# First expert chosen at run time, no slots for empty experts, weight chunks and VectorE steps moved: attention, mixture of experts and a dense layer on one core

## What is computed

```python
# attention: q, k, v (8, 8, 576, 64), p (8, 8, 32, 64)
p_packed = sm_attn(p, k, v)
out = sm_attn(q, p_packed, p_packed)
# mixture of experts: N = 4608 tokens, D = 512, E = 8, F = 1024
logits = x @ w_gate
expert_idx = np.argmax(logits, axis=1)
...
for e in range(E):
    mask = expert_idx == e
    if not mask.any():
        continue
    xe = x[mask]
    h = np.maximum(xe @ w1[e], 0.0)
    ye = h @ w2[e]
    out[mask] = gate_w[mask, None] * ye
# dense: 512 -> 2048 -> 512
h = x @ w_in
r = np.maximum(h, 0.0)
g = s * (r * r) + b
return (g @ w_out).astype(np.float32)
```

## Time and profile before

| | |
|---|---|
| three runs | 1541.33 us median (1539.59 to 1544.24) |
| the profiled execution | 1552.85 us, of which 1551.0 us are the span of its trace |
| PE busy | 1459.8 us (94%) |
| DVE, ACT, POOL busy | 31%, 31%, 27% |
| chain that ended last | PE 91%, DVE 3%, issue 3%, ACT 1%, DMA 1%, POOL 1% |
| 24718 instructions | PE 8664, DVE 811, ACT 973, POOL 275 that count as busy |

### The profile page before, as it was taken

How to read it: one execution, slowest core, us unless ns; L and a number is a source line. 1 busy time by engine, 2 the same in 40 slices (tenths; PEclk the granted TensorE clock), 3 DMA queues, 4 the chain that set the end, 5 groups by cost and what they waited for, 6 DMA issues and landing times.

```text
span 1551.0 us, 24718 instructions
## 1 busy us (share of the span) xinstructions
PE 1459.8 (94%) x8664; PEld 1174.4 (76%) x8665; DVE 475.2 (31%) x811; ACT 479.9 (31%) x973; POOL 413.2 (27%) x275
## 2 busy tenths in 40 slices
PE   6887369999999999998999999999999999999996
PEld 5655358888888888886888888888888888888885
DVE  3777621111111111113523232322323232332322
ACT  5666123333333333332222222222222222222221
POOL 1244578448266557104501010100101010010100
PEclk9899579999999999999999999999999999999998
DMA  9798345234243333212101010100101000000000
GB/s 315 219 273 237 117 152 160 84 108 135 68 142 108 108 122 115 81 47 89 63 14 42 7 41 14 35 13 14 41 7 41 14 34 14 14 27 0 27 1 27
DMA packets 52850, 122.78 MB, mean 79 GB/s; under 512 B 6608, under 2 KB 12752, under 8 KB 52816
## 3 DMA queue, kind: packets, MB, share of 16 engines
q1 hardware_dynamic: 33728, 79.21, 16.8%
q10 hardware_dynamic: 13136, 24.19, 5.0%
q0 software_dynamic: 5952, 18.92, 3.4%
HBM read 90.78 MB, written 31.52 MB: 79 GB/s over the span
## 4 chain that ended last, share of the span: by engine, by line
PE 91%; DVE 3%; issue 3%; ACT 1%; DMA 1%; POOL 1%; another core or an unknown queue 0%; ACTq 0%; DVEq 0%
PE psum L675 18%; PE psum L676 18%; PE psum L677 18%; PE psum L751 8%; PE psum L750 8%; PE psum L749 8%; PE psum L719 2%; PE psum L508 2%; PE psum L684 1%; PE psum L737 1%; PE psum L610 1%; PE psum L548 1%; PE psum L569 1%; PE psum L623 1%; DVE x_rows L1142 1%
## 5 line engine op out<-in xcount | busy, mean ns | idle before, releaser
L1256 DVE SCALAR_TENSOR_TENSOR s_r_r<-r_relu,s_col 128x512 f32<-128x512 f32 x144 | 116.1, 806 | 449.3 <-ACT r_relu L973 449.3
L483 POOL DMA_INDIRECT out_dram<-out_sb,out_row_of_y x36 | 35.6, 989 | 746.9 <-ACT out_sb L983 738.7
L675 PE MATMUL psum<-weights_split,gT_hi 128*128 128x512 f32 x576 | 230.9, 401 | 2.3 <-DVE gT_lo L1258 2.2
L973 ACT ACTIVATE r_relu<-psum 128x512 f32<-128x512 f32 x144 | 86.1, 598 | 470.9 <-PE psum L751 456.2
L676 PE MATMUL psum<-weights_split,gT_hi 128*128 128x512 f32 x576 | 227.7, 395 | 0.0
L677 PE MATMUL psum<-weights_split,gT_lo 128*128 128x512 f32 x576 | 227.7, 395 | 0.0
L751 PE MATMUL psum<-yT_hi,weights_split 128*128 128x512 f32 x576 | 227.3, 395 | 0.0
L749 PE MATMUL psum<-yT_hi,weights_split 128*128 128x512 f32 x576 | 225.7, 392 | 0.0
L750 PE MATMUL psum<-yT_lo,weights_split 128*128 128x512 f32 x576 | 225.5, 392 | 0.0
L396 POOL TENSOR_TENSOR weights_split<-weights_raw,one 128x1024 fp32r<-128x1024 f32 x70 | 135.3, 1933 | 253.6 <-PE psum L677 243.1
L398 POOL TENSOR_TENSOR weights_split<-weights_raw,weights_split 128x1024 fp32r<-128x1024 f32 x70 | 169.6, 2423 | 5.5
(11 more groups left out here) (154 smaller groups left out, 1833.3 us busy)
## 6 DMA issues: line engine op xcount, KB each, us to landing
weights_raw<-in_moe_w_dram SPq DMA_DIRECT2D x64, 512.0 KB
x_slot<-x_by_expert ACTq DMA_DIRECT2D x40, 257.0 KB, 2.7
y_sorted<-y_slot ACTq DMA_DIRECT2D x40, 256.5 KB, 3.2
k_sb<-in_k_dram SPq DMA_DIRECT2D x16, 576.0 KB, 6.4
q_sb<-in_q_dram SPq DMA_DIRECT2D x16, 576.0 KB, 7.6
v_sb<-in_v_dram SPq DMA_DIRECT2D x48, 192.0 KB
y_tile<-y_sorted SPq DMA_DIRECT2D x32, 256.5 KB, 2.6
weights_raw<-in_moe_w_in_dram SPq DMA_DIRECT2D x8, 512.0 KB
```

Of the source, the lines that this page charges most:

```text
L675: nc.tensor.matmul(dst, lhs[0][:, col:col + P], rhs[0], start=first_, stop=False)
L973: nc.scalar.activation(rel[:], ps[:, HFB + par, :], ACT.Relu).then_inc(rel_done, 1)
L1256: nc.vector.scalar_tensor_tensor(sq[par][:], rel[:], s_col[:], rel[:], ALU.mult, ALU.mult).then_inc(sq_done, 1)
```

## The change

It has five parts.

- **First expert.** In unit 5 VectorE takes the expert with the most tokens in batch 0 (`lead_expert`; with these inputs expert 3). Its chunks are the first to be loaded, now in units 10 to 15 and behind the last one, and it comes first in the order of slots.
- **Order and empty experts.** The tables first sort the experts: the chosen one, then the others, and those without tokens last. An empty expert has no slot. There are still eight loads of weights; if experts are empty, the last one with slots is loaded again, and its slots are cut between its loads (`starts`, `expert_of`). With these inputs expert 7's ten slots become 5 and 5. The tables now end in two places: `tables` when rows and slot count are there, `wtables` when the weight tables are.
- **Slot 0.** SyncE issues its load, at row 0 of the chosen expert's region, once batches 0 to 5 are scattered (2 x 96 on `x_sent[0]` and `[1]`, on the other two as `lead_count` says: 96 if the chosen expert has 256 tokens in six batches, and it has 576). Its up projection waits neither for tables nor for the last scatters, and VectorE does its `x_lo` ahead of the tables, its `h_lo` behind both. TensorE does slot 0's down projection ahead of slot 1's up.
- **Scatters.** All scatters of batches 6 and 7 now wait for the last positions. GpSimd splits all eight chunks of the second expert.
- **VectorE's last steps** are written out one by one: the `turn_packs` of the last unit goes ahead of `positions` of batch 6, and `experts` of batch 7 ahead of the last two `out_x`.

```diff
             for u in range(2, UNITS):
                 load_k(u)
                 load_q(u)
-                if u % 2 == 0:
-                    n = u // 2 - 1
-                    chunk(n, n, expert_chunk(0, n))
+                if u == UNITS - NCH + 2:
+                    sp.wait_ge(lead_done, 2)
+                    lead_ = sp.value_load(lead_i[0:1, 0:1], min_val=0, max_val=E - 1)
+                    row = sp.value_load(lead_row[0:1, 0:1], min_val=0, max_val=(E - 1) * REG)
+                if u >= UNITS - NCH + 2:
+                    n = u - (UNITS - NCH + 2)
+                    chunk(n, n, expert_chunk(lead_, n))
                 load_v(u)
...
+            for b in range(XBUFS):
+                sp.wait_ge(x_sent[b], 2 * BATCH_DMA if b < 2 else sent)
+            sp.wait_ge(t0_full, UNITS)
+            sp.wait_ge(t1_full, UNITS)
+            sp.dma_start(xin[:], rows_dram[bass.ds(row, P), :]).then_inc(xin_in, 16)
+            sp.wait_ge(wtables, 1)
+            second = sp.value_load(expert_of[0:1, 1:2], min_val=0, max_val=E - 1)
+            for n in range(EARLY, 2 * NCH):
+                chunk(n % NCH, n, expert_chunk(second, n % NCH))
...
-            for j in range(4, J):
+            pool.wait_ge(pos_done, B)
+            for j in range(J):
                 scatter(B - 2, j)
             for j in range(J):
                 scatter(B - 1, j)
 
             for sent in x_sent:
                 pool.wait_ge(sent, BATCH_DMA * B // XBUFS)
-            pool.wait_ge(conv, EARLY + 2)
-            for n in range(EARLY + 2, 2 * NCH):
+            for n in range(EARLY, 2 * NCH):
                 split(n % NCH, n, WBUF)
...
+            x_hi(0)
+            keep_columns(0, 0)
+            act.wait_ge(need_done, 1)
+            sent = act.value_load(sent_need[0:1, 0:1], min_val=BATCH_DMA, max_val=2 * BATCH_DMA)
+            for b in range(XBUFS):
+                act.wait_ge(x_sent[b], 2 * BATCH_DMA if b < 2 else sent)
             act.wait_ge(tables, 1)
...
             load(1)
             relu(0)
+            h_hi(0)
             x_hi(1)
             keep_columns(1, 1)
+            for sent in x_sent:
+                act.wait_ge(sent, 2 * BATCH_DMA)
             load(2)
...
-            step(nc.vector.tensor_scalar(nslot[0][:, 0, E:], cnt_i[:], 1.0, None, ALU.max))
+            step(nc.vector.tensor_copy(nslot[0][:, 0, E:], cnt_i[:]))
```

301 lines of the change are left out of this document (208 added, 93 removed).

## The result

The changed kernel took **1533.72 us** (median of 6 runs, 1527.77 to 1543.43), the kernel before beside it 1542.78 us (1539.59 to 1550.04). The ratio is 0.9931, 95% interval [0.9907, 0.9954]: faster, by 9 to 10.6 us. Forecast were 1521.7 us, a gain of 19.6 and a range of 1509 to 1531. The direction was right; half of the gain did not arrive, and the time lies above the range.

What follows compares the result with a forecast made beforehand. TensorE was taken to bound the expert stage, plus its waits ahead of it. Terms 12.5 + 7.6 - 0.5 = 19.6 us, off the median 1541.3, gave 1521.7 us; range 1509 to 1531.

Steps and rivals of the forecast that it cites:

- One slot fewer, 12.5 us: Expert stage: the empty expert's slot goes, 39 slots in place of 40, gaining 12.5 us.
- Slot 2's up projection 7.6 us earlier: Turn from attention to experts: slot 0's early start brings slot 2's up projection to 221.8 from 229.36, 7.6 us.
- hole ending at 28.7: After slot 0's up projection: TensorE stands some 8 us for VectorE's tables, until the down projection at 206.1.
- Half of the head start is spent on tables: Slot 0's up projection starts 16.3 us earlier, but after waiting for VectorE's tables only 7.6 remain at slot 2.
- Positions of batch 7: VectorE at the end of attention: reordered last steps make these positions end 1.7 us earlier, at 188.6.
- The gap of 4.1 us: VectorE's unexplained late start at 183.76: kept in the path; by bounds 4.1 us gained or 2.2 lost.
- lead_expert, 0.5 us: Attention stage, unit 5: choosing the expert adds seven small VectorE instructions, taken as 0.5 us lost.
- the moved chunks, 0: Attention stage: moving chunk loads to units 10 to 15 taken as nothing, bounds 2.7 us gained and 5 lost.
- Behind 229 us nothing changes but the count of slots.: Everything after slot 2's up projection, including the dense stage: no change assumed except one slot fewer.
- It does not do what it says: Rival, expert stage: the empty expert keeps a slot, 12.5 us more, 1534 us; chance 0.02.
- The head start is spent altogether: Rival, turn to experts: table chains cost over 7 us more, slot 2 no earlier, 1529 us; chance 0.10.
- Slower: Rival, attention units 10 to 15: chunks on full DMA engines cost 28 us, 1550 us; chance 0.03 over 24 us, 0.02 under.

Runs made afterwards that it cites:

- e1: The changed kernel, unedited, run again for a second profile; ratio to the kernel before 0.9935 [0.9921, 0.9949].
- e13: The changed kernel, unedited, run again in a later session; ratio to the kernel before 0.9945 [0.9930, 0.9960].
- e17: The changed kernel with the head start undone: TensorE waits for the slot tables before slot 0, whose low part comes behind them; ratio to the kernel before 0.9924.
- e5: The kernel before with only yT's tiles and those above them moved up by 32 bytes; ran once, 1543.67 us (kernel before 1544.95).
- e7: The kernel before with every tile moved up by 64 bytes; ran once, 1546.18 us (kernel before 1544.95).
- e10: The kernel before with the first expert's chunks and their roundings as late as in the changed kernel; ratio to the kernel before 0.9991 [0.9977, 1.0005].
- e11: The kernel before with only VectorE's last steps put in the changed kernel's order; ratio to the kernel before 0.9996 [0.9978, 1.0013].
- e8: The changed kernel with its dense tiles moved up by 160 bytes; ran once, 1529.58 us (kernel before 1544.95).
- e9: The changed kernel with dense tiles moved up by 160 bytes and 130 semaphore increments ahead of TensorE's first transposes; ratio to the kernel before 0.9995 [0.9976, 1.0014].
- e12: e9's kernel with relu(0) ahead of the wait for slot tables and h_lo(0) amid the weight tables; ratio to the kernel before 0.9958 [0.9942, 0.9974].
- e18: The changed kernel with dense tiles at the old place, slot 1 in TensorE's loop, 22 semaphore increments, chunks in units 8 to 15; ratio to the kernel before 0.9855.
- e16: The changed kernel with the first expert's chunks loaded as early as in the kernel before, expert 3 written into the code; ratio to the kernel before 0.9930.
- e2: The changed kernel with one 32-byte tile ahead of the dense tiles, putting them at multiples of 64 bytes; ratio to the kernel before 0.9908 [0.9883, 0.9934].
- e6: The kernel before with gT's tiles moved up by 32 bytes and yT's by 128; ran once, 1543.86 us (kernel before 1544.95).
- e3: The kernel before, unedited, run again for a second profile; ratio 1.0002 [0.9990, 1.0013].
- e4: The kernel before with one 32-byte tile ahead of the dense tiles, putting them 32 past a multiple of 64; ratio to the kernel before 1.0032 [1.0016, 1.0049].

## Why the prediction was half right

- **One slot fewer, 12.5 us.** Right: 39 loads, 12.52 us apart.
- **Slot 2's up projection 7.6 us earlier.** Right in size, to 0.1 us: 51.9 us after the last attention matmuls before, 44.25 after; the wider set of profiles has 7.4 (64.1 against 56.7, means up to slot 3). The pieces: first up projection 12.7 us after these matmuls, forecast 12.8, by luck (next point); slot tables 8.2 to 8.6 us, forecast 8; weight tables 5.8, forecast 6 (8.0 in e1 and 7.8 in e13, where VectorE stands some 2 us between its own steps, for a reason that the trace does not show); hole ending at 28.7, forecast 28.7. At 0.18 us a step the upper ends of the two table sums would be 8.5 and 6.3, not 8.8 and 6.6; the values taken do not change. "Half of the head start is spent on tables" was right as well, and e17 makes it sharper: the half ahead of the slot tables is worth nothing.
- **Positions of batch 7.** Forecast 11.2 us after the last attention matmuls began, measured 8.2 (171.51 less 163.27). The gap of 4.1 us that I kept is gone. Where the kernel before has no holds (below) it was not there before either: 8.7 us in e5, and the new order is worth 0.6 there. It did not reach the end: VectorE's tables stand behind the low part of slot 0's rows, and TensorE waited 3.58 us for these rows' load (173.41), so the tables began 12.5 us after the last attention matmuls (175.78), just where the forecast has them: two misses of about 3 us that cancel. Where the load comes earlier (e1, e13) the slot tables begin at 10.0 and 10.1 us, but the weight tables end where they did (26.4 and 26.3, 26.5 in the first profile).
- **lead_expert, 0.5 us, and the moved chunks, 0.** This term was mis-sized: in place of 0.5 the attention part is longer by about 2.4 us in one kind of session and 6 in the other. My bound for the chunks, 5 us lost, nearly takes that in; the value taken, nothing, does not. I had judged by a mean DMA share and by a profile that shows no wait for k, q and v. That profile has holds (below). None of the eleven profiles with holds shows TensorE waiting for k or q from 40 us to the end of the attention part, and all nine without them do, in both kernels: 3.9 us in all in the changed kernel's first profile, 2.6 to 5.4 in e5 to e7, e10 and e11, 3.7 to 9.6 in e8, e9 and e12. Two of these waits, from TensorE's timeline of the changed kernel:

```profile
118.37 1.54 PE L558 MATMUL psum<-ident,k_sb 128*128 128x128 f32 x6 [0.92 <-DMA k_sb<-in_k_dram]
...
141.41 0.52 PE L558 MATMUL psum<-ident,k_sb 128*128 128x128 f32 x3 [1.56 <-DMA q_sb<-in_q_dram]
```

  How much of it is the chunks' place is not settled: e18 points that way by time, e16 hardly (its interval overlaps e13's), e10 does not, in a session without holds.
- **"Behind 229 us nothing changes but the count of slots."** This is the step that failed. It cost 6.7 us: some 5.5 by the tiles' place and 1.2 by the place of the loop's code (the sum of what the three longer groups exceed 91.42 by, 0.9 to 1.4 in five profiles). The sentence argued from the code of the dense stage, which is the same. Its addresses were not, neither those of its data nor its own, and the allocation of both kernels could have been laid side by side beforehand.
- The sum with what was measured is 12.5 + 7.4 - 2.4 - 6.7 = 10.8 us, against 9 to 10.6 by the times. In the sessions with holds it is 12.5 + 7.4 - 6.2 - 6.7 = 7.0 against 8.5 to 10, so 1.5 to 3 us are open there. The sum leaves out one stretch, from the last slot's up projection to the first group's scatter. It takes 123.7 to 123.9 us in the five profiles of the kernel before and its variants with the loop's tiles in place, and 122.9 to 126.7 in the five of the changed kernel with its tiles out of place (126.4 in the first profile, 122.9 in e1), of which 0.7 is the first group's longer period. TensorE waits twice there, and its clock behind these waits explains a part: in the ten microseconds from each of the two restarts the granted clock is 0.83 and 0.83 in the first profile, 1.00 and 1.00 in e1, 0.70 and 0.72 in e2, where the stretch takes 128.3 us. It is not all, for e13 has 1.00 and 0.83 at 126.7 us and the first profile of the kernel before 1.00 and 0.85 at 123.9. So the closeness of the sum to the time is in part chance.
- **The rivals.** "It does not do what it says" gave 1534 us, nearly the measured time, and is refuted by the 39 loads: a right number is no evidence for its mechanism. "The head start is spent altogether" gave 1529; half of it is. "Slower" named one of the two right places, the attention part, at 28 us against 2.4 to 6. None named the dense stage. The range ended at 1531, since it was made of the cases I had thought of.
- The base: the forecast subtracts its gain from the median, which is right. Subtracted from the profiled run it would have read 1533.2, next to the measured time by accident.

## What to carry to other kernels

A change in one stage moves the tiles and the code of all stages behind it. Before saying that the rest stays as it is, lay the addresses of the large tiles and the positions of the large loops of both programs side by side, and fix them: a declared tile of 32 bytes was worth 0.3% here (5.7 us), about half of what the change itself brought. When work is started earlier, ask what the next step waits for: 9 us of head start ended in a hole whose end was set by another engine's chain. And padding is work: measure what one filler costs before putting in 130.

## What the runs showed of the hardware

- **The tiles' place in the dense stage, within 64 bytes.** fp32r matmuls of 128 x 512 follow each other at 0.230 to 0.234 us. With yT's or gT's tiles 32 bytes past a multiple of 64 a group of 384 takes 91.2 to 91.27 us, with both 91.41, with neither 90.73, in all twenty profiles (90.8 in e2 and e8; groups behind a new fetch of the loop are longer). It is not the matmul's own operand that decides (e6, and the slots, whose 12.52 us do not change). Why the 64-byte case saves in the blocks that stream yT only, and in e2 in the other half, is open.
- **Instruction fetches of a loop.** A loop of 1688 TensorE instructions was fetched again in every turn at one place of the code and usually not at others, 126 instructions before it or 129 behind; a turn with fetches costs 0 to 1.4 us. The page of the Trainium skill named above calls crossing a block "mostly hidden"; that agrees with 27 fetches in three turns for 1.2 us in all. My forecast used this sentence to decide that a gap was not code, which held (the same code shows the gap in e3 and e4 and not in e5 to e7), but did not ask what it means for a loop.
- **A semaphore increment on TensorE costs 0.126 us** (130 of them 16.4 us).
- **Holds in the attention part.** In the sessions of the higher level, and in the first profile of the kernel before, ScalarE stands for 2.9 us (3.3 the last time), about every 20 us, released by something that the trace does not show; VectorE mostly stands for 1.0 to 1.7 us beside it. ScalarE's timeline of e3; the same row recurs at 101.32, 121.54 and 141.80, and there is none in e5 to e12:

```profile
81.80 1.50 ACT L808 COPY kqT<-psum 128x768 f32<-128x768 f32 x2 [2.92 <-remote]
```

  Five such holds are 14 us, which is how far the kernel before moves between sessions (1543 and 1557). They come in both kernels, four in e13. One chip showed both levels, in e9 to e12 and in e13 to e16. TensorE works on through most of a hold, to 81.5 in the one shown. From 40 us on a profile has either the holds or waits of TensorE for k and q, never both. What they are is open, and they are why the unexplained gap of the prediction could not be explained from one profile.
